# x moved by 64 bytes in SBUF: a spacer of 64 bytes per partition in place of 128

## The chip, the cores and the metric

One core of one Trainium2 chip runs the whole program. The metric is the device time in microseconds (us), the median of several runs. Engines are named as in the profile: PE is TensorE's matmul side and PEld its weight load, DVE is VectorE, ACT is ScalarE, POOL is GpSimd, SP is SyncE, which issues most DMAs.

## The reference

All values are float32. An attention with capped scores is followed by two MLPs on 896 tokens.

```python
# q, k, v: (2, 12, 448, 64); cap = 30
scores = cap * np.tanh((q @ k.T / np.sqrt(64)) / cap)
attn = np.exp(scores - scores.max(-1)) ; attn = attn / (attn.sum(-1) + 1e-09)
x = (attn @ v) as (896, 768)
# w_in (768, 2048), w_out (2048, 768), one pair for each layer
h = x @ w_in ; x = (np.maximum(h, 0) ** 2) @ w_out      # layer 0
h = x @ w_in ; x = (h / (1 + np.exp(-h))) @ w_out       # layer 1
```

## The kernel before

The attention takes the heads in 12 pairs and ends at about 98 us. It leaves x, with the model dimension on the partitions, as 12 slices of 128 x 448 (6 chunks of the model dimension for each of 2 batches). The rest of the time goes to the two MLPs.

Every MLP product is made of three matmuls in the type float32r. A float32 operand is split into a rounded part (hi) and what is left (lo), and `passes` (lines 552 to 557) adds hi by hi, hi by lo and lo by hi: line 555 loads the weights' hi and streams x_hi or g_hi, line 556 loads the hi again and streams x_lo or g_lo, line 557 loads the weights' lo and streams x_hi or g_hi. Each of them is a weight load of 128 columns and a matmul of 448 columns.

Each layer has two stages on the hidden dimension, and each of these has two parts. `hidden` (line 573) makes 8 tiles of the hidden dimension from x: 6 chunks x 2 batches x 3 passes for each tile. `model` (line 594) makes the output from g, the activated hidden values, by a scheme with 7 products in place of 8 in each of 3 groups: 4 chunks x 3 passes for each product. So the order on TensorE is x, g, x, g for layer 0 and the same again for layer 1. The first two tiles of the very first x part are made by `hidden_first` (line 559), one half of a tile before the last head pair is finished. The last product of all is cut into 256 and 192 columns.

Weights are split while they are used: ScalarE writes the hi part (`tile_high`, line 713, `prod_high`, line 726), VectorE the lo part (`tile_low`, line 965, `prod_low`, line 970), both into w_hl. TensorE waits for the lo part of a tile or product before its first weight load.

x is written in two places. In the attention VectorE's `finish` writes x_hi at line 927 and x_lo at line 932. Between the layers ScalarE copies y into x_hi (line 776) and VectorE subtracts to get x_lo (line 1111). The g values are written by ScalarE at line 765 and VectorE at line 1011.

SBUF is laid out by hand. The long-lived tensors, among them w_hl, stand at the left end, then those of the attention, in whose place g_hi, g_lo and y come later. x_hi and x_lo stand at the right end, behind a spacer, and the output's rows take the same right end later, without a spacer. In each partition w_hl starts at byte 35,936, g_hi at 57,184, g_lo at 107,360, y at 157,536, x_lo at 186,208 and x_hi at 207,712: all of them 96 modulo 256. A slice of x, g or y has 448 x 4 = 1,792 bytes, one of the weights 128 x 4 = 512. The operands that TensorE reads in the attention also start at 96 modulo 256.

Of the kernel before, what the change touches and what calls it, by code (L numbers as in the profile page):

```python
# [13 lines left out]
P = 128  # L14
# [3 lines left out]
def attention_then_two_mlps(nc, q, k, v, cap, w_in1, w_out1, w_in2, w_out2, out):  # L18
# [18 lines left out]
    BL = 32  # L37
# [25 lines left out]
    with ctx:  # L63
# [3 lines left out]
        def sb(stack, name, shape, dt=F32, side=None):  # L67
            return stack.enter_context(nc.sbuf_tensor(name, shape, dt, side=side))
# [47 lines left out]
            u3 = sb(hid, "u3", [P, S])  # L116

        with ExitStack() as act_x:
            sb(act_x, "x_step", [P, BL], side="right")
            x_hi = sb(act_x, "x_hi", [P, B * KC, S], F32R, side="right")  # L120
            x_lo = sb(act_x, "x_lo", [P, B * KC, S], F32R, side="right")
        with ExitStack() as act_o:
# [1171 lines left out]
```

## Time and profile before

| | before |
|---|---|
| median of 3 runs | 538.78 us (538.76 to 538.99) |
| the profiled execution | 544.16 us |
| its span, first to last instruction | 542.4 us |
| mean granted TensorE clock | 0.998 of full |
| PE busy | 532.6 us (98%), 2,628 matmuls |
| PEld busy | 441.2 us (81%), 2,628 weight loads |
| DVE busy | 362.5 us (67%) |
| ACT busy | 261.0 us (48%) |
| POOL busy | 79.8 us (15%) |

The span runs from the first to the last instruction of one profiled execution; its own time is 1.8 us longer, and the runs without a profile are shorter than both. Busy time of PE counts a matmul from its start to its modelled end, and a matmul starts before the one ahead of it has ended, so that a duration in the rows (367 ns) is longer than the distance from one start to the next. In the views, "x384" is the number of instructions in a group; "idle before" is the idle time of the engine just before them and what ended it. Lines are those of the kernel before.

### The profile page before, as it was taken

What the parts mean: (1) busy time and instruction counts of PE and PEld (TensorE: products, weight loads), DVE (VectorE), ACT (ScalarE), POOL (GpSimd) and SP (SyncE); (2) the same over time, 40 slices, a digit from 0 to 9 for tenths busy, and PEclk for the clock granted to TensorE, in tenths of its full rate; (3) what the DMA queues carried; (4) which work ended last, traced back from release to release, by engine and by line L of the source; (5) the groups of instructions that cost most, each with busy time, mean ns of one, the idle gap of its engine ahead of it and who ended that gap; (6) DMA issues with size and microseconds to landing.
All of it is one profiled execution on the core that took longest, in us unless ns stands there. A gap on an engine that the chain in (4) does not pass through costs nothing.

```text
span 542.4 us, 7105 instructions
## 1 busy us (share of the span) xinstructions
PE 532.6 (98%) x2628; PEld 441.2 (81%) x2628; DVE 362.5 (67%) x625; ACT 261.0 (48%) x404; POOL 79.8 (15%) x54
## 2 busy tenths in 40 slices
PE   7999998999999999999999999999999999999996
PEld 5333334799999999999999999999999999999996
DVE  3488887597677734766799744556855255568985
ACT  4999995155444232544434344444433145444230
POOL 1899999100000000000000000000000000000000
PEclk9999999999999999999999999999999999999999
DMA  8799601051202202412022024220220251020546
GB/s 223 196 242 229 166 25 56 3 147 48 79 0 79 58 2 79 117 58 79 0 79 60 0 59 136 59 61 18 78 58 1 59 136 50 9 79 7 119 67 91
DMA packets 82181, 42.17 MB, mean 78 GB/s; under 512 B 26848, under 2 KB 79072, under 8 KB 82144
## 3 DMA queue, kind: packets, MB, share of 16 engines
q1 hardware_dynamic: 77984, 40.32, 28.9%
q10 hardware_dynamic: 4128, 1.38, 1.1%
q8 instruction: 21, 0.34, 0.3%
q14 instruction: 16, 0.13, 0.1%
q0 software_dynamic: 32, 0.00, 0.0%
HBM read 38.93 MB, written 2.75 MB: 77 GB/s over the span
## 4 chain that ended last, share of the span: by engine, by line
PE 89%; ACT 5%; POOL 3%; issue 2%; DVE 0%; POOLq 0%; ACTq 0%
PE banks L555 27%; PE banks L556 27%; PE banks L557 27%; ACT prob L680 3%; PE banks L474 2%; PE banks L467 2%; ACT prob L687 2%; POOL asum L435 1%; PE banks L521 1%; PE banks L495 1%; POOL asum L431 1%; POOL asum L428 1%; PE banks L464 1%; PE banks L486 1%; ACT prob L677 0%
## 5 line engine op out<-in xcount | busy, mean ns | idle before, releaser
L555 PE MATMUL banks<-x_hi,w_hl 128*128 128x448 f32 x384 | 141.0, 367 | 0.0
L556 PE MATMUL banks<-x_lo,w_hl 128*128 128x448 f32 x384 | 140.8, 367 | 0.0
L557 PE MATMUL banks<-x_hi,w_hl 128*128 128x448 f32 x384 | 140.8, 367 | 0.0
L557 PE MATMUL banks<-g_hi,w_hl 128*128 128x448 f32 (+1 forms) x340 | 124.1, 365 | 0.0
L556 PE MATMUL banks<-g_lo,w_hl 128*128 128x448 f32 (+1 forms) x340 | 124.1, 365 | 0.0
L555 PE MATMUL banks<-g_hi,w_hl 128*128 128x448 f32 (+1 forms) x340 | 124.1, 365 | 0.0
L555 PEld LDWEIGHTS banks<-x_hi,w_hl 128*128 128x128 f32 x384 | 72.1, 188 | 7.9 <-issue 1.4
L556 PEld LDWEIGHTS banks<-x_lo,w_hl 128*128 128x128 f32 x384 | 72.1, 188 | 6.5
L557 PEld LDWEIGHTS banks<-x_hi,w_hl 128*128 128x128 f32 x384 | 72.1, 188 | 6.4
L965 DVE TENSOR_TENSOR w_hl<-w_raw,w_hl 128x768 fp32r<-128x768 f32 x32 | 31.5, 985 | 58.6 <-ACT w_hl L713 58.5
L746 ACT ACTIVATE work<-banks 128x448 f32<-128x448 f32 x64 | 31.3, 542 | 78.3 <-PE banks L557 69.3
L555 PEld LDWEIGHTS banks<-g_hi,w_hl 128*128 128x128 f32 x340 | 63.9, 188 | 5.9
L556 PEld LDWEIGHTS banks<-g_lo,w_hl 128*128 128x128 f32 x340 | 63.9, 188 | 5.9
L557 PEld LDWEIGHTS banks<-g_hi,w_hl 128*128 128x128 f32 x340 | 63.9, 188 | 5.8
L726 ACT ACTIVATE w_hl<-w_raw 128x512 fp32r<-128x512 f32 x60 | 37.4, 627 | 45.7 <-PE banks L557 43.8
L765 ACT ACTIVATE g_hi<-work 128x448 fp32r<-128x448 f32 x80 | 43.1, 573 | 27.4 <-DVE work L1032 21.5
L970 DVE TENSOR_TENSOR w_hl<-w_raw,w_hl 128x512 fp32r<-128x512 f32 x60 | 40.9, 687 | 21.6 <-ACT w_hl L726 20.5
L1011 DVE TENSOR_TENSOR g_lo<-work,g_hi 128x448 fp32r<-128x448 f32 x80 | 48.3, 620 | 6.5 <-ACT g_hi L765 5.2
L765 ACT ACTIVATE g_hi<-t_sum 128x448 fp32r<-128x448 f32 x32 | 18.5, 579 | 48.0 <-DVE t_sum L1023 24.5
L687 ACT ACTIVATE prob<-prob,cap_a 128x1792 f32<-128x1792 f32 (+1 forms) x24 | 38.5, 1603 | 0.8
L1004 DVE TENSOR_TENSOR work<-work 128x448 f32<-128x448 f32 x32 | 18.6, 622 | 28.0 <-ACT work L746 28.0
L680 ACT ACTIVATE prob<-banks,qk_scale 128x896 f32<-128x896 f32 x36 | 34.6, 994 | 3.2 <-PE banks L467 3.2
(67 smaller groups left out, 528.0 us busy)
## 6 DMA issues: line engine op xcount, KB each, us to landing
w_raw<-in_moe_w_in_dram SPq DMA_DIRECT2D x32, 384.0 KB, 3.4
w_raw<-in_moe_w_out_dram SPq DMA_DIRECT2D x24, 512.0 KB, 5.2
qk_raw<-in_k_dram SPq DMA_DIRECT2D x44, 112.0 KB, 3.0
qk_raw<-in_q_dram SPq DMA_DIRECT2D x44, 112.0 KB, 3.3
v_t<-in_v_dram SPq DMA_DIRECT2D x24, 96.0 KB, 2.8
out_dram<-rows SPq DMA_DIRECT2D x38, 56.0 KB, 2.2
qk_raw<-in_k_dram ACTq DMA_DIRECT2D x4, 112.0 KB, 3.1
qk_raw<-in_q_dram ACTq DMA_DIRECT2D x4, 112.0 KB, 4.2
```

The source lines that it names most:

```text
L555: pe.matmul(dst, hi[:, kk, :], mov_hi, start=start, stop=False, skip_group_check=onto)
L556: pe.matmul(dst, hi[:, kk, :], mov_lo, start=False, stop=False, skip_group_check=onto)
L557: return pe.matmul(dst, lo[:, kk, :], mov_hi, start=False, stop=stop, skip_group_check=onto)
L680: act.activation(chunk_of(j, u), banks[:, score_bank(j, u):score_bank(j, u) + 2, 0:S], ACT.Tanh, scale=qk_scale[:, 0:1]).then_inc(s_ring, 1)
L687: act.activation(t, t, ACT.Exp, scale=cap_a[:, 0:1]).then_inc(s_exp, 1)
L726: act.activation(prod_split(g, n)[0], prod_source(g, n), ACT.Copy).then_inc(s_w_hi, 1)
L746: act.activation(work[2 * (p % 2) + b][:, :], ring[2 * (p % 2) + b][:, 0:S], ACT.Relu if layer == 0 else ACT.Silu).then_inc(s_h[layer], 1)
L765: act.activation(g_hi[:, q, i, :], g_source(q)[:, :], ACT.Copy).then_inc(s_g_hi, 1)
L965: dve.tensor_tensor(lo, tile_raw(p), hi.bitcast(F32), ALU.subtract).then_inc(s_w_lo, 1)
L970: dve.tensor_tensor(lo, prod_source(g, n), hi.bitcast(F32), ALU.subtract).then_inc(s_w_lo, 1)
L1004: dve.tensor_tensor(w[:, :], w[:, :], w[:, :], ALU.mult).then_inc(s_square, 1)
L1011: dve.tensor_tensor(g_lo[:, q, i, :], g_source(q)[:, :], g_hi[:, q, i, :].bitcast(F32), ALU.subtract).then_inc(s_g, 1)
```

## The change

The spacer x_step, a tensor that nothing reads or writes, has 16 float32 values in each partition in place of 32, that is 64 bytes in place of 128. x_hi and x_lo, which are placed to the left of it from the right end, start 64 bytes further right: x_hi at 207,776 and x_lo at 186,272, both 160 modulo 256. Everything else keeps its address, and no instruction, wait or order changes.

```diff
         with ExitStack() as act_x:
-            sb(act_x, "x_step", [P, BL], side="right")
+            sb(act_x, "x_step", [P, BL // 2], side="right")
             x_hi = sb(act_x, "x_hi", [P, B * KC, S], F32R, side="right")
             x_lo = sb(act_x, "x_lo", [P, B * KC, S], F32R, side="right")
```

## Rows read from the trace of the kernel before

**Rows 1.** The page's busy time by engine (share, count) and clock in 40 slices.

```profile
PE 532.6 (98%) x2628; PEld 441.2 (81%) x2628; DVE 362.5 (67%) x625; ACT 261.0 (48%) x404; POOL 79.8 (15%) x54
...
PEclk9999999999999999999999999999999999999999
```

**Rows 2.** The page's chain that ended last: shares of the span.

```profile
PE 89%; ACT 5%; POOL 3%; issue 2%; DVE 0%; POOLq 0%; ACTq 0%
PE banks L555 27%; PE banks L556 27%; PE banks L557 27%; ACT prob L680 3%; PE banks L474 2%; PE banks L467 2%; ACT prob L687 2%; POOL asum L435 1%; PE banks L521 1%; PE banks L495 1%; POOL asum L431 1%; POOL asum L428 1%; PE banks L464 1%; PE banks L486 1%; ACT prob L677 0%
```

**Rows 3.** Groups of PE instructions by line and shape: busy us, mean ns.

```profile
L555 PE MATMUL banks<-x_hi,w_hl 128*128 128x448 f32 x384 | 141.0, 367 | 0.0
...
L555 PE MATMUL banks<-g_hi,w_hl 128*128 128x448 f32 x332 | 121.9, 367 | 0.0
```

**Rows 4.** Timeline of PE, the first matmul of each part: start us, duration us.

```profile
98.39 0.47 PE L555 MATMUL banks<-x_hi,w_hl 128*128 128x448 f32 x1
...
153.21 0.36 PE L555 MATMUL banks<-g_hi,w_hl 128*128 128x448 f32 x1
...
204.28 0.36 PE L555 MATMUL banks<-x_hi,w_hl 128*128 128x448 f32 x1
...
262.65 0.36 PE L555 MATMUL banks<-g_hi,w_hl 128*128 128x448 f32 x1
...
314.44 0.37 PE L555 MATMUL banks<-x_hi,w_hl 128*128 128x448 f32 x1
...
373.96 0.37 PE L555 MATMUL banks<-g_hi,w_hl 128*128 128x448 f32 x1
...
426.04 0.37 PE L555 MATMUL banks<-x_hi,w_hl 128*128 128x448 f32 x1
```

**Rows 5.** Waits from 98 to 540 us, TensorE's only row: us, times, longest.

```profile
PEld banks L555 <- issue: 0.7, 1, 0.7
```

**Rows 6.** Timeline of matmuls and weight loads from 276.2 to 278.1 us.

```profile
276.23 0.36 PE L556 MATMUL banks<-g_lo,w_hl 128*128 128x448 f32 x1
276.42 0.37 PE L557 MATMUL banks<-g_hi,w_hl 128*128 128x448 f32 x1
...
277.04 0.37 PE L557 MATMUL banks<-g_hi,w_hl 128*128 128x448 f32 x1
...
277.07 0.19 PEld L555 LDWEIGHTS banks<-g_hi,w_hl 128*128 128x128 f32 x1
...
277.44 0.37 PE L556 MATMUL banks<-g_lo,w_hl 128*128 128x448 f32 x1
277.45 0.19 PEld L557 LDWEIGHTS banks<-g_hi,w_hl 128*128 128x128 f32 x1
...
278.06 0.37 PE L556 MATMUL banks<-g_lo,w_hl 128*128 128x448 f32 x1
```

**Rows 7.** Timeline of the end: matmuls of 256 columns, and the last one.

```profile
536.35 0.28 PE L556 MATMUL banks<-g_lo,w_hl 128*128 128x256 f32 x1
...
536.47 0.28 PE L557 MATMUL banks<-g_hi,w_hl 128*128 128x256 f32 x1
...
537.80 0.27 PE L557 MATMUL banks<-g_hi,w_hl 128*128 128x192 f32 x1
```

**Rows 8.** By line, writers of x and g: busy us, mean ns; a line's waiters.

```profile
L1011 DVE TENSOR_TENSOR g_lo<-work,g_hi 128x448 fp32r<-128x448 f32 x80 | 48.3, 620 | 6.5 <-ACT g_hi L765 5.2
...
L932 DVE TENSOR_TENSOR x_lo<-banks,x_hi 128x448 fp32r<-128x448 f32 x12 | 7.5, 625 | 1.2
L927 DVE TENSOR_TENSOR x_hi<-banks,rinv 128x448 fp32r<-128x448 f32 x12 | 7.5, 625 | 4.8 <-PE banks L486 4.5
...
L1111 DVE TENSOR_TENSOR x_lo<-y,x_hi 128x448 fp32r<-128x448 f32 x12 | 7.1, 618 | 0.0
...
L776 ACT ACTIVATE x_hi<-y 128x448 fp32r<-128x448 f32 x12 | 6.7, 572 | 5.0 <-DVE y L1050 4.9
...
  PEld banks L474: 2.6, 4
```

## The prediction

> **What bounds the kernel now.** I first read busy time by engine and the granted clock [rows 1]. TensorE (PE) is busy for 532.6 of the 542.4 us span, VectorE for 362.5, ScalarE for 261.0. The clock is granted in full, the 2.4 GHz level, in every slice of the span. Next comes the chain of work that ended last [rows 2]: TensorE holds 89% of it, and 81% belongs to three lines, 555 to 557, the matmuls of the two MLPs. So the question is the tempo of these matmuls. Their groups [rows 3] show 1,152 that stream x (three times 384) and 1,020 that stream g, with 367 ns for a full-width one of either kind. That duration is no tempo: a matmul overlaps the next one. What counts is the distance from start to start, and for that I took the first matmul of each stage from the timeline [rows 4].
>
> A stage on x holds 8 tiles x 6 chunks x 2 batches x 3 passes = 288 matmuls; a stage on g holds 3 groups x 7 products x 4 chunks x 3 passes = 252. The second x stage starts at 204.28 and the g stage after it at 262.65: 58.37 us / 288 = 202.7 ns. The g stage before it gives (204.28 - 153.21) / 252 = 202.7 ns. In the second layer the same work is slower: x from 314.44 to 373.96, 59.52 / 288 = 206.7 ns; g from 373.96 to 426.04, 52.08 / 252 = 206.7 ns. There is no idle time behind either tempo: from 98 us on TensorE's waits hold a single row, 0.7 us of a weight load that waited for nothing the profile shows [rows 5]. So this kernel has two tempos, 4.0 ns apart, both at full clock and both met by x and by g.
>
> Where the tempo changes can be seen in the timeline of matmuls and weight loads about 277 us [rows 6]. Each weight load (188 ns, 0.19 in the rows) normally starts with the matmul ahead of the one that needs it, as at 277.44 and 277.45. The load beside the matmul of 277.04 started at 277.07, some 30 ns late. Until then the starts are 0.20 to 0.21 apart, from then on always 0.206 to 0.207 (three in 0.62 us), and the fast tempo never comes back: 4 stage starts later the tempo is still 206.7. The tempo is thus a lock between the stream of the moving operand and the load of the next weights, which run side by side, and a disturbance of 30 ns is enough to knock it over. If one column goes in each cycle of 2.4 GHz, an estimate that the 0.12 us at 256 columns [rows 7] bears out, 448 columns take 186.7 ns, and 16.0 ns are lost at the fast tempo and 20.0 ns at the slow one. The narrow matmuls of the end [rows 7] show that the load's own 188 ns does not set the tempo: at 256 columns the starts are 0.12 us apart, so loads follow each other more closely than that when they may. It is the stream that is longer than its columns, by 13 ns at 256 and by 16 to 20 at 448.
>
> **The change, part by part.** It adds no instruction and removes none. x_hi and x_lo, the two halves of x, move 64 bytes towards the right end in all partitions. Before, both start at 96 modulo 256, as do w_hl (the weights), g_hi, g_lo and y; after, at 160. Each slice of x is 1,792 bytes = 7 x 256 and each slice of weights is 512 = 2 x 256, so every x matmul has its two operands at a distance of 0 modulo 256 before and 64 after. g matmuls stay at 0.
>
> Writers and readers of x other than TensorE: VectorE writes x_hi and x_lo in the attention and x_lo between the layers, ScalarE copies x_hi [rows 8]. These are 12 + 12 + 12 + 12 instructions of 572 to 625 ns. I cost them at nothing. Between the layers no instruction had line 1111 or 776 as what it waited for. In the attention TensorE waited 2.6 us in 4 cases for line 932 [rows 8], and that chain is set by the twelve writes' full 625 ns; a change of 5% in one (31 ns) would be 0.37 us over all twelve even if nothing hid it. The output tiles that later lie over x have a place of their own that the spacer does not move. The line that subtracts two SBUF operands into g_lo needs 620 ns [rows 8], that of x_lo 618: no room for a large gain either.
>
> The x matmuls are the only term. The trace has no pair of operands at a distance of 64, since all weights and moving operands that TensorE reads lie at distance 0 here. I bound the price by the nearest rows, the tempos at distance 0. From below: the fast pattern has shorter and longer steps in it, of which the shortest is 0.19 to 0.20 us (276.23 to 276.42 [rows 6]); 1,152 x matmuls at 200 ns, half of which now take 202.7 and half 206.7 (mean 204.7), would save 4.7 x 1,152 = 5.4 us. From above: one more step of 4.0 ns over the slow tempo for each x matmul, from a mean of 204.7 to 210.7, is 6.0 x 1,152 = 6.9 us, and with the g matmuls of the first layer pulled along another 2.0 as below, together near 9 us. A full loss of the overlap, 188 ns for each load, would be 217 us; the narrow matmuls show that loads pipeline, so I leave it out.
>
> The value that I take: the slow tempo throughout. Reasons in the rows: the fast tempo was inherited by every stage from the one before it, across the boundaries at 153.21, 204.28 and 262.65, without a break. With x at another distance from the weights than g, the lock has to survive six changes of the distance instead of none, and a single late load cost it for good. The slow tempo, on the other hand, held for 1,258 full-width matmuls. So 882 matmuls of lines 555 to 557, from 98.39 to 277.2 us, go from 202.7 to 206.7: 882 x 4.0 = 3.5 us. Of these 558 are x (270 + 288) and 324 are g: 2.2 and 1.3 us. Nothing hides it, as TensorE has no idle time there. The tail after the last matmul, from 537.80 on [rows 7], moves with it and keeps its length.
>
> Against the profiled execution this gives 544.16 + 3.5 = 547.7 us. The median of the runs is 538.78, 5.4 us under the profiled execution. The slow stretch of the profile costs 1,258 x 4.0 = 5.0 us, so it may be that an unprofiled run keeps the fast tempo to the end; then the loss would be up to 2,140 x 4.0 = 8.6 us if all turn slow and 4.6 if the x matmuls alone do. I take the 3.5 us of the profile, which lies between the smallest of these losses (2.2, x alone as in the profile) and the largest: 538.78 + 3.5 = 542.3 us.
>
> A rule speaks against any effect. The Trainium skill, on the page "SBUF — State Buffer", section "Who interferes with whom", says that PE and ACT never wait on anyone, and "TensorE: Matmul & The Clock Gate", section "Step-by-step: what each phase is for", that loading the next weights takes no read bandwidth from the running matmul. By that the distance could not matter and the time would be 538.8. The trace agrees only in part: its load and matmul do overlap, but the second page's section "Back-to-back issue gap" gives N/2.4 + 2.5, 189.2 ns for 448 columns, and the rows have 202.7 and 206.7.
>
> **The rivals.**
>
> *No effect.* The tempo depends on the moment at which a load starts, not on addresses. For it: the slices of x and g alternate between 0 and 256 modulo 512 while the slices of weights don't, and the slow tempo is three starts in 0.62 us whatever the chunk [rows 6], so a distance of 256 certainly costs nothing; and x and g, at very different places of SBUF, share both tempos. Against it: nothing in the trace has a distance of 64. Time: 538.8 us.
>
> *The distance frees the stream (faster).* The 16 to 20 ns that a stream loses are collisions of the moving reads with the weight reads. Both start at the same moment from the same place modulo 256, which could be the worst case. Two sizes: the x matmuls that are slow now regain the fast tempo, 576 x 4.0 = 2.3 us, 536.5 us; or all x matmuls reach 200 ns, 5.4 us, 533.4 us. It decides if the x stages come out under 202.7 ns. For it: the loss exists and grows with the stream. Against it: it grew under a changed moment, not a changed address.
>
> *The distance costs a step of its own (slower still).* x matmuls at 210.7 ns, or the timed runs losing a fast tempo they held throughout: 538.78 + 6.9 = 545.7, and with the g matmuls up to 538.78 + 8.6 or 9 = 547 to 548 us.
>
> **How the numbers follow.** Chances: x or all matmuls slow by the steps seen (541.0 to 543.5) 0.35; slower still (543.5 to 549) 0.17; no effect, within 0.2% 0.30; faster 0.18 (0.11 near 536.5, 0.07 below 535.5). What a measurement of this kernel can tell from no change is about 0.2%, 1.1 us. So slower 0.52, same 0.30, faster 0.18. The forecast is the likeliest single case of the first group, 542.3. The range leaves out the deep gain (0.07) and the far end of the losses (0.04 above 548), and some of the gain near 536: 536.0 to 548.0. The likeliest case alone would have 541.0 to 543.5.
>
> **What would show it right or wrong.** The start-to-start distances by stage, taken as above: x stages (288 matmuls) and g stages (252). Right: x at 206 to 207 ns in all four stages, and g with it; the busy time of other engines, the counts and the granted clock unchanged. If x is slow and g fast, the lock is remade at each boundary and only the x term is right. If both show 202.7 in the first layer, the distance does nothing; if the change of tempo comes earlier or later than 277 us with x unchanged before it, the cause is the moment of a late load and not the address. x under 202 would prove the rival of the freed stream, x over 208 the step of its own. Any change in the length of the attention before 98 us would mean that I was wrong to price the writers at nothing.

## The result and the profile after

The change made the kernel faster: 535.88 us in the median (535.18 to 536.25 in 12 runs) against 539.05 us, and the ratio of the means is 0.9928, with a 95% interval of 0.9907 to 0.995. A second series gave 535.89 us against 538.84, a ratio of 0.9944 (0.993 to 0.9958). I had forecast 542.3 us and a range from 536.0, so both the direction and the range were missed.

The 43 recorded runs of the kernel before lie between 538.6 and 539.7 us (32) or 5 us above, between 543.5 and 544.2 (10, the profiled one with 544.16 among them), and one is at 540.4, which stays unexplained. Of the changed kernel's 17 runs none is above 536.3.

The page of the changed kernel: the span, busy time by engine (share, count) and the clock in 40 slices. They answer [rows 1].

```profile
span 533.4 us, 7105 instructions
...
PE 523.3 (98%) x2628; PEld 439.9 (82%) x2628; DVE 362.3 (68%) x625; ACT 261.2 (49%) x404; POOL 79.7 (15%) x54
...
PEclk9999999999999999999999999999999999999999
```

Counts and clock are as before, and VectorE and ScalarE are busy for the same time to 0.2 us. TensorE is busy for 9.3 us less and the span is 9.0 us shorter. The timeline of the changed kernel, the first matmul of each part and at the end the last matmul of all (start us, duration us), answers [rows 4].

```profile
97.39 0.47 PE L555 MATMUL banks<-x_hi,w_hl 128*128 128x448 f32 x1
...
151.51 0.36 PE L555 MATMUL banks<-g_hi,w_hl 128*128 128x448 f32 x1
...
202.58 0.36 PE L555 MATMUL banks<-x_hi,w_hl 128*128 128x448 f32 x1
...
260.19 0.36 PE L555 MATMUL banks<-g_hi,w_hl 128*128 128x448 f32 x1
...
311.26 0.36 PE L555 MATMUL banks<-x_hi,w_hl 128*128 128x448 f32 x1
...
368.86 0.36 PE L555 MATMUL banks<-g_hi,w_hl 128*128 128x448 f32 x1
...
419.93 0.37 PE L555 MATMUL banks<-x_hi,w_hl 128*128 128x448 f32 x1
...
477.54 0.36 PE L555 MATMUL banks<-g_hi,w_hl 128*128 128x448 f32 x1
...
528.83 0.27 PE L557 MATMUL banks<-g_hi,w_hl 128*128 128x192 f32 x1
```

The x parts: (260.19 - 202.58) / 288 = 200.0 ns, (368.86 - 311.26) / 288 = 200.0, (477.54 - 419.93) / 288 = 200.0. The g parts: (202.58 - 151.51) / 252 = 202.7, (311.26 - 260.19) / 252 = 202.7, (419.93 - 368.86) / 252 = 202.7. So x has a tempo (the mean distance from one start to the next) that the kernel before never showed, g keeps the fast one, and the slow one, 206.7, is gone.

That accounts for all of the 9.0 us between the two profiled spans. x at 200.0 in place of 202.7 is worth 2.67 ns x 1,134 (the 18 x matmuls ahead of 98 us belong to another stretch) = 3.0 us. The slow stretch of the kernel before cost 1,248 x 4.0 = 5.0 us (the trace has 1,248 full-width matmuls from 277.2 us on, not the 1,258 of the prediction). The last 1.0 us is the start of the part after the attention, 98.39 against 97.39. That one is not the change's: in the profiles of this study the first x matmul of all starts anywhere from 89.4 to 90.4 us, whatever the distance (90.3 before, 89.4 after, 90.2 in e14, which is the changed kernel again). No run of the kernel before near 539 us has a trace, but 544.16 less the 5.0 us of the slow stretch is 539.2, so I take these runs for ones that kept the fast tempo. Against them only the 3.0 us should count, and the measured difference of medians in the second series is 538.84 - 535.89 = 2.95.

### The profile page after: what moved, and what is told of

It is laid out like the page before. It is cut to its first block, busy times and chain, and to the rows that moved or that the text cites. A ratio compares the mean times of both kernels' runs of the same rounds, so it can differ in the third digit from the quotient of the medians.

```text
span 533.4 us, 7105 instructions
## 1 busy us (share of the span) xinstructions
PE 523.3 (98%) x2628; PEld 439.9 (82%) x2628; DVE 362.3 (68%) x625; ACT 261.2 (49%) x404; POOL 79.7 (15%) x54
## 4 chain that ended last, share of the span: by engine, by line
PE 88%; POOL 5%; ACT 3%; issue 1%; DMA 1%; DVE 0%; ACTq 0%; POOLq 0%
PE banks L557 27%; PE banks L555 27%; PE banks L556 27%; PE banks L474 3%; PE banks L467 2%; POOL asum L435 2%; POOL asum L431 2%; ACT prob L687 2%; ACT prob L680 2%; POOL asum L428 2%; PE banks L495 1%; DMA qk_raw<-in_q_dram 1%; PE banks L464 1%; PE banks L486 1%; ACTq L657 0%
## 5 line engine op out<-in xcount | busy, mean ns | idle before, releaser
L557 PE MATMUL banks<-x_hi,w_hl 128*128 128x448 f32 x384 | 139.4, 363 | 0.0
L556 PE MATMUL banks<-x_lo,w_hl 128*128 128x448 f32 x384 | 139.0, 362 | 0.0
L555 PE MATMUL banks<-x_hi,w_hl 128*128 128x448 f32 x384 | 138.7, 361 | 0.0
```

Of the source, the lines that this page charges most:

```text
L555: pe.matmul(dst, hi[:, kk, :], mov_hi, start=start, stop=False, skip_group_check=onto)
L556: pe.matmul(dst, hi[:, kk, :], mov_lo, start=False, stop=False, skip_group_check=onto)
L557: return pe.matmul(dst, lo[:, kk, :], mov_hi, start=False, stop=stop, skip_group_check=onto)
```

## The experiments

Theory A: each distance between the moving operand and the weights, modulo 256, has a tempo of its own. Theory B: only the moment at which a load starts counts, or else the place of x alone. "Distance" always means the moving operand's start less the weights', modulo 256. In each case the tempo is (start of the next part - start of this one) / 288 for x or / 252 for g. Edits are made to the kernel before unless it is said otherwise.

**e1, the weights are moved and x is not.**

```diff
+        sb(ctx, "w_step", [P, 48])
         w_hl = sb(ctx, "w_hl", [P, 6 * KQ * P], F32R)
+        sb(ctx, "w_rest", [P, 16])
```

> Edit: x keeps the spacer of 128 bytes; the weights w_hl are moved instead, by a pad of 192 bytes ahead of them and one of 64 behind, so that both x and g lie 64 bytes above the weights modulo 256, and every tensor other than w_hl keeps its place modulo 256. Theory A (the start-to-start distance of MLP matmuls depends on the distance of the moving operand from the weights modulo 256; at 64 it is 200.0 ns, at 0 it is 202.7 or 206.7): x and g stages both at 200.0 ns in all eight parts, so another 1,000 x 2.7 = 2.7 us below the changed kernel, 539.05 - 5.9 = 533.2 us. Theory B (where x itself stands in its partition matters, or merely that the addresses changed): x back at 202.7 ns, g unchanged or no pattern, 538 to 539 us, with the slow tempo possible again.

Measured: 533.53 us (533.17 to 533.68 in 4 runs), ratio 0.988 (0.983 to 0.9931). The first matmuls of three parts in its timeline; two lines more in the file make line 555 line 557:

```profile
202.61 0.36 PE L557 MATMUL banks<-x_hi,w_hl 128*128 128x448 f32 x1
...
260.21 0.36 PE L557 MATMUL banks<-g_hi,w_hl 128*128 128x448 f32 x1
...
310.80 0.36 PE L557 MATMUL banks<-x_hi,w_hl 128*128 128x448 f32 x1
```

x: 57.60 / 288 = 200.0 ns; g: 50.59 / 252 = 200.8; the g part after it, from 368.40 to 418.80, has 50.40 / 252 = 200.0. The g part with 200.8 has two longer steps, at 274.41 and 274.64, and this time the profile names what TensorE's weight load waited for (in brackets), VectorE's lo part of the weights:

```profile
274.41 0.37 PE L559 MATMUL banks<-g_hi,w_hl 128*128 128x448 f32 x1
...
274.64 0.19 PEld L557 LDWEIGHTS banks<-g_hi,w_hl 128*128 128x128 f32 x1 [0.24 <-DVE w_hl L972]
274.64 0.47 PE L557 MATMUL banks<-g_hi,w_hl 128*128 128x448 f32 x1
...
274.95 0.36 PE L558 MATMUL banks<-g_lo,w_hl 128*128 128x448 f32 x1
```

Behind this wait the tempo is 200.0 again. x is where it was before the change and has the changed kernel's tempo. So it is not x's own place that counts, but its distance from the weights, and g obeys it too. Theory B's second half falls; e2 to e5 and e8 speak against its first.

**e2 to e5, other distances for x.** The spacer is left out (e2), or has 48 (e3), 8 (e4) or 56 values (e5) in place of 32. The edit of e3:

```diff
-            sb(act_x, "x_step", [P, BL], side="right")
+            sb(act_x, "x_step", [P, 48], side="right")
```

> Edit: no spacer, x lies 128 bytes above the weights modulo 256, g at 0. Theory A with a period of 256: a tempo of its own for x, anywhere from 199 to 210 ns, the same in all four x stages; g at 202.7. Theory A with a period of 128: x as at distance 0, 202.7 ns. Theory B: any x stage between 200 and 207, with no steady value.

> Edit: spacer of 192 bytes, x lies 192 bytes above the weights modulo 256, that is 64 below; g at 0. Theory A: a steady tempo of its own. If only the size of the distance matters, 200.0 ns as at +64; if the sign matters, because the stream that starts behind catches the other up, another value, above 202.7 and up to 210 ns. Theory B: no steady value.

> Edit: spacer of 32 bytes, x lies 96 bytes above the weights modulo 256; g at 0. Theory A: between the tempo at 64 (200.0 ns) and that at 128 (the run beside this one); if the tempo falls the further apart the streams are, below 200.0. Theory B: no steady value.

> Edit: spacer of 224 bytes, x lies 160 bytes above the weights modulo 256, g at 0. Theory A (each distance modulo 256 has a tempo of its own): x steady in all four stages, between those at 128 (203.9 ns, run e2) and 192 (202.2 ns, run e3), about 203; g at 202.7 or 206.7. Theory B (addresses do not matter): x at 202.7 or 206.7 as g.

Measured once each: 542.08, 542.25, 543.31 and 535.91 us. In e4's timeline an x part starts at 206.11 and ends at 265.24:

```profile
206.11 0.36 PE L555 MATMUL banks<-x_hi,w_hl 128*128 128x448 f32 x1
...
265.24 0.36 PE L555 MATMUL banks<-g_hi,w_hl 128*128 128x448 f32 x1
```

59.13 / 288 = 205.3 ns. In the same way e2 has 58.74 / 288 = 204.0, e3 58.24 / 288 = 202.2 and e5 57.61 / 288 = 200.0. In each run the x parts after the first agree with each other within 0.1 ns. The values are far from a smooth curve: 96 is slower than 64 and than 128, and my expectations of "between its neighbours" missed for e4 and for e5. In e3 every g part, still at distance 0, ran at 206.7, in e5 every one at 202.7. In e2 and e4 it was mixed: behind the same x tempo g ran at 206.6 in its first part, then at 202.7 twice, and in its last part at 206.6 in e2 and at 202.7 in e4. So a g part can come out of an x part in either tempo, and the distance of x alone does not settle which. In e3 the slow g parts cost 996 x 4.0 = 4.0 us, and its x parts gained only 0.5 us (0.5 ns x 1,134).

**e6, x_lo alone at 64.**

```diff
             x_hi = sb(act_x, "x_hi", [P, B * KC, S], F32R, side="right")
+            sb(act_x, "lo_step", [P, 48], side="right")
```

> Edit: x_hi stays at distance 0, x_lo alone lies 64 bytes above the weights modulo 256 (a spacer of 192 bytes between the two). Of three matmuls one streams x_lo. Theory A, each matmul for itself (its stream collides with the load that runs beside it): a start-to-start mean in x of about 201.8 ns if the others keep 202.7, with the gain behind the x_lo matmuls alone. Rival A2: the tempo is a lock of the whole sequence, and mixed distances break it: x at or above 203 ns, or 206.7. Theory B: 202.7 until something knocks it over.

Measured: 540.08 us, and in the timeline x from 204.30 to 262.96, 58.66 / 288 = 203.7 ns, above the 202.7 of distance 0. Improving one operand of three made the sequence slower. The tempo belongs to the sequence (A2), not to each matmul for itself.

**e7 and e8, eight cuts, at distance 0 and at 64.** In tiles 2 and 5 of each x part one matmul is cut into 256 and 192 columns, in e8 in the kernel of e1:

```diff
+                    if p in (2, 5) and n == B:
+                        cut_passes(ring[2 * (p % 2) + b][:, 0:S], tile_split(p), kk,
+                                   x_hi[:, b * KC + kk, :], x_lo[:, b * KC + kk, :])
+                        continue
```

> Edit: the kernel before, with one x matmul in tiles 2 and 5 of each of the four x parts cut into 256 and 192 columns, which computes the same and shifts the moment of every start behind it: eight disturbances, each costing some 25 to 40 ns by itself. Theory A: at distance 0 there are two tempos, and a disturbance can change which one holds: after some of the eight the tempo goes from 202.7 to 206.7 ns or back, in steps that begin at a cut. Rival: the change at 277 us had another cause (power, the clock, the work of other engines), and the eight cuts change nothing, 202.7 before some moment and 206.7 after it.

> Edit: the same eight cuts in the kernel whose weights were moved (run e1), x and g at distance 64. Theory A: at 64 there is a single tempo, 200.0 ns, and it comes back after each cut. Rival: 64 has a slow tempo too, which nothing has provoked so far; one of the cuts brings it out, and the stretch behind it is above 202 ns.

Measured: 541.95 and 533.7 us. The timeline of e7 around its cut at 132.00 ("x2" are the two pieces):

```profile
131.39 0.36 PE L555 MATMUL banks<-x_hi,w_hl 128*128 128x448 f32 x1
131.60 0.36 PE L556 MATMUL banks<-x_lo,w_hl 128*128 128x448 f32 x1
131.80 0.36 PE L557 MATMUL banks<-x_hi,w_hl 128*128 128x448 f32 x1
132.00 0.37 PE L563 MATMUL banks<-x_hi,w_hl 128*128 128x256 f32 x2
...
132.44 0.37 PE L565 MATMUL banks<-x_hi,w_hl 128*128 128x448 f32 x1
132.65 0.37 PE L555 MATMUL banks<-x_hi,w_hl 128*128 128x448 f32 x1
132.85 0.37 PE L556 MATMUL banks<-x_lo,w_hl 128*128 128x448 f32 x1
133.06 0.37 PE L557 MATMUL banks<-x_hi,w_hl 128*128 128x448 f32 x1
```

Ahead of the cut the starts are 0.20 to 0.21 apart, behind it three take 0.62 us, the slow tempo. It held through the whole g part that followed and until the cut at 221.31, which brought the fast one back; the cut at 462.23 brought the slow one again, and the other five left the fast tempo alone. So of seven cuts in the fast tempo two brought the slow one, and the only cut in the slow tempo ended it. A cut costs some 30 ns by itself: in e8 an x part with two of them takes 57.66 us, 0.06 more than in e1. A disturbance of this size can set the tempo, in either direction.

The one at 277 us in [rows 6] came from another engine. VectorE writes the lo part of the weights, line 970, and the product whose first load started late needs it:

```profile
276.34 1.28 DVE L970 TENSOR_TENSOR w_hl<-w_raw,w_hl 128x512 fp32r<-128x512 f32 x2
```

The row holds two writes that overlap. The first ends at 277.02, and the load starts 54 ns after that, at 277.07. The same 52 to 54 ns lie between the write's end and the load in all 20 places, in twelve traces, where the first load of a product came 30 ns or more late. Eight of them are at this product with g at distance 0 in the fast tempo (before, after, e2, e4 to e7, e14), with the load 37 to 51 ns behind the start of the matmul beside it. Only in the kernel before, where it was the 37, did the slow tempo follow. That the upper runs of the kernel before are so alike, 5 us above the lower, fits a tempo that turns at this one place in each of them (1,248 x 4.0 = 5.0), but only one of them has a trace.

In e8 the same cut at distance 64:

```profile
131.79 0.37 PE L565 MATMUL banks<-x_hi,w_hl 128*128 128x256 f32 x2
...
132.43 0.36 PE L557 MATMUL banks<-x_hi,w_hl 128*128 128x448 f32 x1
132.63 0.36 PE L558 MATMUL banks<-x_lo,w_hl 128*128 128x448 f32 x1
132.83 0.36 PE L559 MATMUL banks<-x_hi,w_hl 128*128 128x448 f32 x1
133.03 0.36 PE L557 MATMUL banks<-x_hi,w_hl 128*128 128x448 f32 x1
```

Three starts in 0.60 us at once, and so after all eight cuts. Distance 64 has shown one tempo only.

**e9, x on the other side modulo 512, g at 160.** The spacer has 80 values, and `sb(hid, "g_step", [P, 40])` stands ahead of g_hi.

> Edit: the spacer of x is 320 bytes, so x lies at 64 modulo 256 again but on the other side modulo 512 from the changed kernel; g_hi, g_lo and y are moved by 160 bytes, so g lies at 160. Theory A (distance modulo 256, the same table for x and g; x at 160 had 200.0 ns in run e5): both at 200.0 ns in all parts, 533.2 to 533.7 us as in e1. Rival: the period is 512 or more, or the table belongs to x alone; then x or g leaves 200.0 and the time is above 534.5 us.

Measured: 533.15 to 538.83 us in 10 runs, median 537.46, ratio 0.9911 (0.987 to 0.9952). Its profiled execution is the longest:

```profile
370.55 0.36 PE L556 MATMUL banks<-g_hi,w_hl 128*128 128x448 f32 x1
...
422.62 0.36 PE L556 MATMUL banks<-x_hi,w_hl 128*128 128x448 f32 x1
...
480.23 0.36 PE L556 MATMUL banks<-g_hi,w_hl 128*128 128x448 f32 x1
```

x: 57.61 / 288 = 200.0 ns, so the period of 256 holds. g: 52.07 / 252 = 206.6 ns here, while the x parts of e5 had 200.0 at the same distance. Distance 160 has two tempos like distance 0, 200.0 and 206.6. Both stand in the first g part of this trace:

```profile
166.25 0.36 PE L557 MATMUL banks<-g_lo,w_hl 128*128 128x448 f32 x1
...
166.45 0.36 PE L558 MATMUL banks<-g_hi,w_hl 128*128 128x448 f32 x1
...
166.56 0.19 PEld L556 LDWEIGHTS banks<-g_hi,w_hl 128*128 128x128 f32 x1
166.65 0.38 PE L556 MATMUL banks<-g_hi,w_hl 128*128 128x448 f32 x1
...
166.87 0.37 PE L557 MATMUL banks<-g_lo,w_hl 128*128 128x448 f32 x1
...
167.08 0.37 PE L558 MATMUL banks<-g_hi,w_hl 128*128 128x448 f32 x1
167.28 0.37 PE L556 MATMUL banks<-g_hi,w_hl 128*128 128x448 f32 x1
167.49 0.37 PE L557 MATMUL banks<-g_lo,w_hl 128*128 128x448 f32 x1
```

Up to 166.45 the starts are 0.20 apart, from 166.87 three take 0.62 us. Between them stands a load that started 0.10 us late, 54 ns after VectorE had written its weights' lo part. In the second g part such a load at 285.6 brings the slow tempo, while one at 275.9 had left the fast one. So 802 full-width g matmuls were slow, and 802 x 6.6 ns = 5.3 us is most of the 5.7 us between the longest and the shortest run. My expectation missed here, since one run of e5 had shown one of the two.

**e10 to e12, four more distances.** x and g are set apart by pads and, for 16 bytes, by slices that start 4 values into a larger tensor.

> Edit: x at 32 and g at 224 bytes above the weights modulo 256. Theory A: each a steady tempo of its own, from 200 to 206 ns; so far 0: 202.7 or 206.7, 64: 200.0, 96: 205.3, 128: 204.0, 160: 200.0, 192: 202.2. If the tempo is a smooth function of the distance, 32 and 224 lie between their neighbours, 32 in 200.0 to 202.7 and 224 near 202.5. Rival (it is the sequence of phases, not a function of distance): above both neighbours.

> Edit: x at 48 and g at 80 bytes above the weights modulo 256, by slices that start 16 bytes into their tensors. Theory A with 200.0 ns as a floor (what is left above 186.7 ns has another cause): no tempo under 200.0; 48 at 200 to 202, 80 at 200 to 205. Rival (the best distance lies between the ones tried, and the whole 13 ns are collisions): one of the two clearly under 200.0.

> Edit: x at 176 and g at 144 bytes above the weights modulo 256. With 200.0 ns as a floor: 144 between 200.0 and 204.0, 176 between 200.0 and 202.2. Rival: one of them clearly under 200.0.

Measured: 545.0, 539.64 and 544.39 us, and by the starts of their parts 206.6 ns at 32 (59.51 / 288), 204.4 at 224 (51.52 / 252), 203.0 at 48 (58.45 / 288), 203.3 at 80 (51.24 / 252), 204.2 at 176 (58.80 / 288) and 206.5 at 144 (52.05 / 252). Nothing is under 200.0. All distances together (those other than 0, 64 and 160 come from one profiled run each, so that a second tempo there may not have shown, as it had not at 160 in e5):

| distance, bytes | 0 | 32 | 48 | 64 | 80 | 96 | 128 | 144 | 160 | 176 | 192 | 224 |
|---|---|---|---|---|---|---|---|---|---|---|---|---|
| ns from start to start | 202.7 or 206.7 | 206.6 | 203.0 | 200.0 | 203.3 | 205.3 | 204.0 | 206.5 | 200.0 or 206.6 | 204.2 | 202.2 | 204.4 |

**e13, cuts in the changed kernel, in g too.** The changed kernel with the eight cuts of e7 and eight more in the third product of groups 0 and 1.

> Edit: the changed kernel (x at 64, g at 0) with one matmul cut into 256 and 192 columns in x tiles 2 and 5 of each part, and in g in the third product of groups 0 and 1 of each part: eight cuts in x, eight in g. Theory A: in x the tempo is 200.0 ns again after each cut; in g some cuts bring the slow tempo, 206.7 ns, up to the next cut or the end of that g part, and the x part behind it is at 200.0 ns whatever came before, so that no slow stretch outlives its g part. Time between 535.5 and 538. Rival: g is fast by nature once x is at 64, and no cut in g brings 206.7; then 535.5 to 536.5.

Measured: 536.75 us. The timeline from the second cut in g, and of the boundary to the next x part:

```profile
174.61 0.37 PE L563 MATMUL banks<-g_hi,w_hl 128*128 128x256 f32 x2
...
175.05 0.37 PE L565 MATMUL banks<-g_hi,w_hl 128*128 128x448 f32 x1
175.25 0.37 PE L555 MATMUL banks<-g_hi,w_hl 128*128 128x448 f32 x1
175.46 0.37 PE L556 MATMUL banks<-g_lo,w_hl 128*128 128x448 f32 x1
175.67 0.37 PE L557 MATMUL banks<-g_hi,w_hl 128*128 128x448 f32 x1
...
203.57 0.37 PE L557 MATMUL banks<-g_hi,w_hl 128*128 128x448 f32 x1
203.78 0.36 PE L555 MATMUL banks<-x_hi,w_hl 128*128 128x448 f32 x1
203.98 0.36 PE L556 MATMUL banks<-x_lo,w_hl 128*128 128x448 f32 x1
204.18 0.36 PE L557 MATMUL banks<-x_hi,w_hl 128*128 128x448 f32 x1
204.37 0.36 PE L555 MATMUL banks<-x_hi,w_hl 128*128 128x448 f32 x1
```

One of the eight cuts in g, at 174.6, brought the slow tempo, and it lasted to the end of that g part; the other seven left the fast one alone. With the first x matmuls the steps are 0.20, 0.20 and 0.19, and the g part behind starts at 261.43, (261.43 - 203.78) = 57.65 us later, two cuts included. The next g part is fast. So g at distance 0 can still turn slow in the changed kernel. The x part at 64 ended it here, the only case on record, and all twelve g parts behind such an x part began in the fast tempo (after, e13, e14). In the trace of before the slow tempo ran to the end of the kernel.

**e14 and e15, side by side.** The changed kernel and that of e1, five rounds on one chip.

> The changed kernel itself, on the same chip as e15 and the kernel before. 535.2 to 536.3 us, 3.0 us below the lower cluster of the kernel before (538.6 to 539.4): 1,134 x matmuls x 2.67 ns = 3.0.

> The kernel of e1 (x and g at 64 by moving the weights). 533.2 to 533.7 us in every run: below e14 by the g matmuls, 1,008 x 2.67 ns = 2.7 us, and no second cluster, since distance 64 has shown a single tempo. Rival: 64 has a slow tempo that has been rare so far; then a run or two of some ten at 536 us or more.

Measured: 535.89 us (535.61 to 536.28), ratio 0.9944 (0.993 to 0.9958), and 533.38 us (533.26 to 533.47), ratio 0.9899 (0.9883 to 0.9914); the kernel before had 538.61 to 539.38 in these nine runs. The kernel with all operands at 64 beats both, the kernel before by 5.5 us and the changed one by 2.5; 996 x 2.67 = 2.7 us is what the full-width g matmuls give against the latter, less some 0.2 us of waits for VectorE as in e1. Its eight runs in two series lie within 0.5 us.

## Why the prediction was wrong

*What bounds the kernel.* Right: the matmuls of the MLPs, by their distance from start to start, without idle time. The two tempos, their 4.0 ns and the power of a disturbance of 30 ns are confirmed by e7. What I did not see is that the load at 277 us had waited for VectorE's line 970. The slow stretch had 1,248 matmuls and not 1,258, which changes no term by more than 0.1 us.

*The writers of x cost nothing.* Right. The attention before 98 us did come out 1.0 us shorter, which I had named as a sign against this, but its end moves by 0.8 us between two profiles of the changed kernel itself (97.39 in the first, 98.20 in e14), and the writers themselves take as long as before. Lines 932 and 1111 take 625 and 620 ns in the changed kernel (625 and 618 in [rows 8]):

```profile
L932 DVE TENSOR_TENSOR x_lo<-banks,x_hi 128x448 fp32r<-128x448 f32 x12 | 7.5, 625 | 1.2
...
L1111 DVE TENSOR_TENSOR x_lo<-y,x_hi 128x448 fp32r<-128x448 f32 x12 | 7.1, 620 | 0.0
```

*The value that I took for the x matmuls.* This is the step that failed. I took the two tempos of distance 0 for the only ones, and asked which of them distance 64 would choose. It has one of its own, 200.0 ns. The term of the sum, 882 x 4.0 = 3.5 us of loss, became a gain of 1,134 x 2.67 = 3.0 us on x and nothing on g. From the long life of the slow tempo I concluded that six changes of distance would end in it. With x at 64 no g part began in it, and the one slow stretch was ended by x (e13); only at 192 (e3) did it go as I had thought. The reason given, that the slow tempo is the stable one, had one disturbance in one trace behind it; of fifteen cuts in the fast tempo of distance 0 three brought the slow one (e7, e13), and the one cut in the slow tempo ended it.

*The rival of the freed stream.* It was the right one, its deciding mark (x under 202.7 ns) was met, and its second size had 200 ns in it. But the size was worked out on the profiled execution, where half of the x matmuls were slow, and then taken off a median whose runs mostly are not: 4.7 x 1,152 = 5.4 us where 2.67 x 1,134 = 3.0 us was due. I had seen this in the text ("an unprofiled run keeps the fast tempo to the end") and used it only for the losses. 538.78 - 3.0 would have been 535.8. With a chance of 0.18 for all that was faster, the range stopped at 536.0, 0.1 us short of the result; had it reached a little lower, it would have held the time by luck, with the direction still wrong.

*The reason against it,* that the loss had grown with a changed moment and not with a changed address, was no evidence, since no pair in the trace had another distance. Both count.

*A distance of 256 costs nothing.* Right: e9 has x at 320 and the tempo of 64.

*The rule by which nothing waits.* The Trainium skill, "SBUF — State Buffer", section "Who interferes with whom", says that PE and ACT never wait on anyone. From that I had an unchanged time, and the runs disagree: moving nothing but the weights, by 192 bytes, took 5.5 us off (e15), and 2.67 ns on 2,130 start-to-start distances of TensorE are 5.7 us. Whether TensorE waits for a read there is not shown.

*What stays open.* That stream and load disturb each other in their reads is what the table of distances suggests, as the tempo depends on the difference of two addresses (e1 against the changed kernel). No run had a stream without a load beside it, so it was not shown, nor was where the remaining 13.3 ns go by which 200.0 exceeds my estimate of 186.7. Nor is it known why one late load or cut changes the tempo and the next does not. Why the table is so rough, with 205.3 at 96 and 200.0 at 64, is open as well.

## What to carry to other kernels

Where TensorE is busy without a gap, read the start-to-start distance of its matmuls part by part, not their duration. If one shape shows two values, look at the start of moving operand and weights modulo 256, try a few distances by means of a spacer, and profile each more than once, because a distance can have two tempos. Look too for weight loads that start late at the moment the tempo changes, and for the engine whose write ended just before. A gain read off one profiled execution must be taken off runs in the same tempo.

## What the runs showed of the hardware

- At full granted clock a float32r matmul of 448 columns with its weight load took 200.0 to 206.7 ns from start to start, a span of 3.3%, by the distance of its operands modulo 256 and, at 0 and 160, by what went before.
- Distances 0 and 160 have two tempos each (202.7 and 206.7; 200.0 and 206.6). A disturbance of 30 ns can switch at distance 0 in both directions, and the tempo then held for up to 1,248 matmuls (before). Distance 64 showed one through 16 cuts (e8, e13) and nine waits for VectorE (e1, e8, e15), and its 25 timed runs give no sign of a second.
- A weight load that waited for VectorE's write started 52 to 54 ns after the write's end, in 20 places of twelve traces.
- The tempo is that of the sequence: with x_lo alone moved to 64 it rose to 203.7 (e6).
- Which tempo of distance 0 a g part gets differs with the x part ahead of it: behind x at 192 it was the slow one four times of four (e3), behind 160 (e5) and 64 (after, e13, e14) the fast one each time, behind 128 (e2) each twice, behind 96 (e4) the slow one once of four.
